# A third PSUM buffer while the pipeline fills, and 512-column products read in 16-column blocks from four 512-byte rows in turn

## What is computed

```python
kv_pool = kv.reshape(B, H // r, r, W // r, r, C).mean(axis=(2, 4))     # B=2, H=384, W=32, C=128, r=4
k = v = kv_pool.reshape(B, -1, C) @ w_sr                               # 768 keys
a = softmax(q @ k.T / sqrt(C))                                         # q: 2 x 12288 x 128
x = a @ v                                                              # attention's output, 24576 rows of 128
h = x @ w1_in;  x = (h * cos(h)) @ w1_out                              # first network, d_ff = 2048
h = x @ w2_in;  x = (h * sigmoid(1.702 * h)) @ w2_out                  # second network, d_ff = 2048
```

## Time and profile before

| | us |
|---|---|
| median of 3 runs | 2718.85 (2718.63 to 2722.79) |
| the profiled execution, its own time | 2722.88 |
| its span, first to last instruction | 2721.1 |
| TensorE (PE) busy | 2670.1 (98%) |
| VectorE (DVE) busy | 2097.1 (77%) |
| GpSimd (POOL) busy | 2029.3 (75%) |
| ScalarE (ACT) busy | 1916.3 (70%) |
| mean granted TensorE clock | 0.993 of 2.4 GHz |

### The profile page before, as it was taken

The page is one execution under the profiler, slowest core; times in us unless marked ns, Lnnn a source line. Parts: engine busy times, 40 slices in busy tenths (PEclk is TensorE's granted clock), DMA queues, the critical chain, the costliest instruction groups (busy, mean ns, idle before and its releaser), DMA issues.

```text
span 2721.1 us, 42506 instructions
## 1 busy us (share of the span) xinstructions
PE 2670.1 (98%) x13342; PEld 2263.0 (83%) x13342; DVE 2097.1 (77%) x2761; ACT 1916.3 (70%) x2471; POOL 2029.3 (75%) x1908
## 2 busy tenths in 40 slices
PE   7999999988999999999999999999999999999998
PEld 7999999966888888888888888888888888888886
DVE  6888888855777777777777777777777777777774
ACT  4777777755777777777777777777777777677775
POOL 2887677547878787778778787777878787777873
PEclk9999999988999999999999999999999999999999
DMA  7323222200000000000000000000000000000000
GB/s 191 72 49 81 71 49 50 50 16 8 10 14 15 8 15 8 15 8 15 13 10 15 8 15 8 15 8 15 15 8 15 8 15 8 15 8 15 16 4 12
DMA packets 220707, 67.64 MB, mean 25 GB/s; under 512 B 204544, under 2 KB 204672, under 8 KB 219776
## 3 DMA queue, kind: packets, MB, share of 16 engines
q1 hardware_dynamic: 220672, 67.21, 10.9%
HBM read 42.01 MB, written 25.17 MB: 25 GB/s over the span
## 4 chain that ended last, share of the span: by engine, by line
PE 96%; DVE 2%; ACT 1%; SPq 0%; DMA 0%; issue 0%; POOL 0%; ACTq 0%
PE psum L548 31%; PE psum L549 30%; PE psum L550 30%; PE psum L672 5%; DVE g L1006 0%; DVE g L1014 0%; ACT turns L835 0%; DMA kv_all<-in_kv 0%; SPq L333 0%; ACT g_hi L845 0%; DVE g_lo L1019 0%; DVE neg_max L926 0%; ACT g L847 0%; PE psum L629 0%; DVE kv_all L892 0%
## 5 line engine op out<-in xcount | busy, mean ns | idle before, releaser
L533 POOL TENSOR_TENSOR g_lo<-g,g_hi 128x512 fp32r<-128x512 f32 x768 | 1122.1, 1461 | 91.0 <-ACT g_hi L852 30.3
L1019 DVE TENSOR_TENSOR g_lo<-g,g_hi 128x1024 fp32r<-128x1024 f32 x384 | 598.3, 1558 | 438.0 <-ACT g L847 432.6
L530 POOL CAST g_hi<-g 128x512 fp32r<-128x512 f32 x758 | 535.1, 706 | 365.2 <-DVE g L1014 365.2
L845 ACT ACTIVATE g_hi<-psum 128x1024 fp32r<-128x1024 f32 x384 | 395.8, 1031 | 440.1 <-PE psum L550 440.1
L548 PE MATMUL psum<-x_hi,w_lo 128*128 128x512 f32 x1536 | 605.2, 394 | 21.1 <-DVE g L1014 21.1
L548 PE MATMUL psum<-g_hi,w_lo 128*128 128x512 f32 x1536 | 600.5, 391 | 9.2 <-DVE x_lo L1025 4.2
L550 PE MATMUL psum<-x_hi,w_hi 128*128 128x512 f32 x1536 | 601.2, 391 | 0.0
L549 PE MATMUL psum<-x_lo,w_hi 128*128 128x512 f32 x1536 | 600.7, 391 | 0.0
L549 PE MATMUL psum<-g_lo,w_hi 128*128 128x512 f32 x1536 | 599.2, 390 | 0.0
L550 PE MATMUL psum<-g_hi,w_hi 128*128 128x512 f32 x1536 | 598.9, 390 | 0.0
L1006 DVE SCALAR_TENSOR_TENSOR g<-turns,psum 128x1024 f32<-128x1024 int32 x384 | 463.0, 1206 | 40.7 <-ACT turns L835 40.7
(11 more groups left out here) (74 smaller groups left out, 3039.0 us busy)
## 6 DMA issues: line engine op xcount, KB each, us to landing
q_blocks<-in_q SPq DMA_DIRECT2D x192, 64.0 KB, 2.2
x_dram<-x_out SPq DMA_DIRECT2D x48, 256.0 KB, 2.3
x_raw<-x_dram SPq DMA_DIRECT2D x48, 256.0 KB, 2.8
out<-y_blocks SPq DMA_DIRECT2D x192, 64.0 KB, 2.3
kv_all<-in_kv SPq DMA_DIRECT2D x4, 1536.0 KB, 11.0
kv_all<-in_kv SPq DMA_DIRECT2D x5, 1024.0 KB, 7.1
w_raw<-in_moe_w_in SPq DMA_DIRECT2D x2, 1024.0 KB, 6.9
kv_all<-in_kv SPq DMA_DIRECT2D x2, 512.0 KB, 9.2
```

What stands on the lines that cost most here:

```text
L530: nc.gpsimd.tensor_copy(g1_hi[p % 4][:, t], g1[p % 4][:, t]).then_inc(g1_hi_ready, 1)
L533: nc.gpsimd.tensor_tensor(g1_lo[p % 4][:, t], g1[p % 4][:, t], g1_hi[p % 4][:, t].bitcast(F32), ALU.subtract).then_inc(g1_lo_ready, 1)
L845: nc.scalar.activation(g2_hi[p % 2][:, :], h2[buffer2(j)], ACT.Silu, scale=GELU)
L1019: nc.vector.tensor_tensor(g2_lo[p % 2][:, :], g2[p % 2][:, :], g2_hi[p % 2][:, :].bitcast(F32), ALU.subtract).then_inc(g2_lo_ready, 1)
```

## The change

It has two parts.

1. **A third `h1` buffer in the filling.** `h1` gets banks 4-5 as a third buffer. For steps below 12 the buffer is `s % 3`, and `up1(s)` waits for `multiply(s - 3)`; from step 12 on it is two buffers as before. `up2(0)`, the first to use banks 4-5 for the second network, now waits until all 12 steps of the filling are multiplied. `BY_SCALAR` becomes 1, 2, 4, 5, 7, 8, 10: ScalarE rounds seven steps of the filling where it rounded five.
2. **The order of the columns in the first network's products.** `up1` and `down1` stream their 512 columns as 8 blocks x 4 rows x 16 columns: 16 columns from each of four rows that lie 128 columns (512 bytes) apart, then the next 16 of each. Output columns in PSUM go the same way, so every number lands where it did. The tiles that are streamed (`x1_*`, `g1_*`) begin 384 bytes behind a multiple of 512 (`APART`), while the weights still begin at a multiple of 512. The second network's and attention's products and places stay as they were.

```diff
     LINE = 512
-    BY_SCALAR = [1, 3, 5, 7, 9]
+    STEP = 16
+    APART = LINE - LINE // 4
+    BY_SCALAR = [1, 2, 4, 5, 7, 8, 10]
...
-    def put(name, shape, dt):
+    def put(name, shape, dt, at=0):
         size = 4 * math.prod(shape[1:])
         if size >= LINE:
-            place[0] += -place[0] % LINE
+            place[0] += (at - place[0]) % LINE
...
-        g1.append(put(f"g1_{n}", [P, PAIR], F32))
+        g1.append(put(f"g1_{n}", [P, PAIR], F32, APART))
...
-    h1 = [banks(0, PAIR), banks(2, PAIR)]
+    h1 = [banks(0, PAIR), banks(2, PAIR), banks(4, PAIR)]
...
+    def buffer1(s, p):
+
+        return s % 3 if isinstance(s, int) and s < UP2 else p % 2
...
+            def by_column_block(x):
+
+                return x.rearrange("p (r b e) -> p b r e", b=LINE // (4 * STEP), e=STEP)
+
+            def product_by_block(dst, w_hi, w_lo, x_hi, x_lo, start, stop):
+
+                return product(by_column_block(dst), w_hi, w_lo, by_column_block(x_hi),
+                               by_column_block(x_lo), start, stop)
+
             def up1(s, p, c):
...
-                if not (isinstance(s, int) and s < 2):
+                if not (isinstance(s, int) and s < UP2):
                     pe.wait_ge(g1_ready, s * 2 - 2)
-                n = p // PAIRS % 2
+                elif s >= 3:
+                    pe.wait_ge(g1_ready, s * 2 - 4)
+                n, at = p // PAIRS % 2, buffer1(s, p)
...
-                    last = product(h1[p % 2][:, k * TOK:(k + 1) * TOK], w1_in_hi[:, f:f + P],
+                    last = product_by_block(h1[at][:, k * TOK:(k + 1) * TOK], w1_in_hi[:, f:f + P],
...
-                    last = product(y1_ps, w1_out_hi[:, f, :], w1_out_lo[:, f, :],
+                    last = product_by_block(y1_ps, w1_out_hi[:, f, :], w1_out_lo[:, f, :],
...
-                elif not (isinstance(j, int) and j == 0):
+                elif isinstance(j, int) and j == 0:
+                    pe.wait_ge(g1_ready, 2 * UP2)
+                else:
                     pe.wait_ge(g2_ready, j)
```

More of the change, by code:

```diff
@@ L137, in attention_and_networks @@
         g1_at = place[0]
-        g1.append(put(f"g1_{n}", [P, PAIR], F32))
+        g1.append(put(f"g1_{n}", [P, PAIR], F32, APART))
         place[0] = g1_at
-        g1_lo.append(put(f"g1_lo{n}", [P, PAIR], F32R))
+        g1_lo.append(put(f"g1_lo{n}", [P, PAIR], F32R, APART))
         place[0] = g1_at
-        turns.append(put(f"turns{n}", [P, PAIR], I32))
-        g1_hi.append(put(f"g1_hi{n}", [P, PAIR], F32R))
+        turns.append(put(f"turns{n}", [P, PAIR], I32, APART))
+        g1_hi.append(put(f"g1_hi{n}", [P, PAIR], F32R, APART))
     x1_raw, x1_lo, x1_hi = [], [], []
@@ L146, in attention_and_networks @@
         x1_at = place[0]
-        x1_raw.append(put(f"x1_raw{n}", [P, TOK], F32))
+        x1_raw.append(put(f"x1_raw{n}", [P, TOK], F32, APART))
         place[0] = x1_at
-        x1_lo.append(put(f"x1_lo{n}", [P, TOK], F32R))
-        x1_hi.append(put(f"x1_hi{n}", [P, TOK], F32R))
+        x1_lo.append(put(f"x1_lo{n}", [P, TOK], F32R, APART))
+        x1_hi.append(put(f"x1_hi{n}", [P, TOK], F32R, APART))
     assert place[0] <= kv_end
@@ L834, in count_turns @@
                 act.wait_ge(h1_ready, i + 1)
-                nc.scalar.activation(turns[p % 4][:, :], h1[p % 2], ACT.Copy, bias=0.25,
+                nc.scalar.activation(turns[p % 4][:, :], h1[buffer1(i, p)], ACT.Copy, bias=0.25,
                                      scale=1.0 / (2 * math.pi)).then_inc(turns_ready, 1)
@@ L1006, in reduce_angle @@
                 nc.vector.scalar_tensor_tensor(g1[p % 4][:, :], turns[p % 4][:, :], -2 * math.pi,
-                                               h1[p % 2], ALU.mult,
+                                               h1[buffer1(i, p)], ALU.mult,
                                                ALU.add).then_inc(angle_ready, 1)
@@ L1013, in multiply @@
                     t = slice(k * TOK, (k + 1) * TOK)
-                    nc.vector.tensor_tensor(g1[p % 4][:, t], h1[p % 2][:, t], g1[p % 4][:, t],
+                    nc.vector.tensor_tensor(g1[p % 4][:, t], h1[buffer1(i, p)][:, t], g1[p % 4][:, t],
                                             ALU.mult).then_inc(g1_ready, 1)
```

## The result

The changed kernel takes 2745.31 us, median of four runs (2744.78 to 2746.19), against 2718.74 for the kernel before in the same comparison: a ratio of 1.0095 (95% interval 1.0078 to 1.0113, written in brackets from here on), slower by 27 us in the medians. The profiled execution took 2746.19, its span is 2744.3.

The account below looks back on a forecast made before the run. The prediction took TensorE's matmul price to bound the steady pipeline and waits the filling. Its terms, -21 (third buffer), -49 (column order) and +4 (second network), sum to -66, from 2718.85 to 2653 us; range 2641 to 2706.

Parts of the forecast that it names:

- What bounds the kernel: Steady pipeline: TensorE busy 500 of 500 us, so a matmul's price is the kernel's; in the filling a wait ends last.
- Part 1, -21 us: Filling: the third buffer removes waits for `multiply`, so `up1(12)` starts earlier; -21 us, bounds -15 (less 1 or 2) to -26.
- that sum: Filling: `up1(12)` starts at 581.1 + 9 x 4.3 = 619.8 us, against 643.5, with two half-clock stretches allowed for.
- Part 2, -49 + 4 us: Steady stretch: new column order makes 4482 first-network matmuls 11 ns cheaper, -49 us; +4 for the second network's disturbed spacing.
- if positions within 512 bytes are what collides, nothing collides any more: First network: stream and weight load stay 384 to about 128 bytes apart in the 512-byte line, never zero.
- the extra of 13.3: Steady pipeline: a 512-column matmul takes 226.7 ns against 213.3 at full clock; the 13.3 ns was called no fixed charge.
- looks like something two reads fight over: TensorE: the matmul's extra 13.3 ns was put on its stream and the next matmul's weight load meeting.
- 11 of 13.3: First network's matmuls: 11 ns of the extra taken as saved, nearest the half-clock rows, leaving 2.
- The bound of +24 us: Part 2's worst side: extra of 19 ns, from 232 ns after a hiccup, over 4482 matmuls; range -60 to +24 us.
- The second network, +4: Its 4608 matmuls keep 226.7 ns, but losing the rhythm costs 25 ns in each of 372 slots: 9 us, half taken.
- Slower: Rival, every `up1` and `down1`: 31 jumps a matmul at one cycle each, 12.9 ns, +58 us, total 2756; chance 0.14.
- The milder form of it: Rival, first network: matmuls stay at 232 ns, +24 - 21, about no change; chance 0.04 for cancelling part 1.

Follow-up runs that it names:

- two rows: Against the changed kernel: first network's streams in 16-column blocks taken in turn from two rows 1024 bytes apart, offset 128 bytes; 2776.89 us (2774.84 at offset 0, 2767.31 at 192).
- the faster pace: Against the changed kernel, with offset 0: first network's columns in two passes, all even blocks of 4 columns, then the odd ones; 2726.20 us.
- the two fine rows: Against the run with two rows 1024 bytes apart: blocks of 4 columns (16 bytes) in place of 16; 2805.48 us.

## Why the prediction was wrong

It gave 2653 us (2641 to 2706); it is 2745. Point by point:

- **What bounds the kernel: right.** A matmul's price in the steady pipeline is the kernel's price; 5 ns on it became some 44 us.
- **Part 1, -21 us: right in the mechanism, the exact figure with some luck.** `up1(2)` at 577.96 (forecast 578), GpSimd's `g_lo` as the main releaser, clock 0.95. `up1(12)` came at 621.6 (forecast 619.8 plus 2 for cold stretches), but not by that sum: the slots took 4.0 us and not 4.3, and the last one 8.5, with the wait of 4.2 us for the first split of the second network's `x`, which the sum left out though the trace of before has it, and with the one cold stretch that was left. The two errors nearly cancel. The run with the buffer alone put part 1 at -19 in its span, and in the filling at -21.2.
- **Part 2, -49 + 4 us: wrong in sign, +42** (the change against the buffer alone; 44 us longer in the steady pipeline, with attention some 1.5 us shorter in this execution). The first network's matmuls went from 226.7 to 235.1 ns, not to 216. The step that failed is "if positions within 512 bytes are what collides, nothing collides any more". Three things in it didn't hold. The places repeat every 256 bytes (offset 256 equals offset 0 in two orders), so the distance of 384 falling to 128 passes through a meeting. But the second thing weighs more: with the period put right, an order meant to keep the reads apart does not help (240 ns at offsets of 0, 128 and 192). That speaks against the extra being the time in which two reads meet, as far as the load goes at the estimated pace of two cycles a column. And the third: the contiguous order was not the costly case that I took it for but as good as any tried. Contiguous or in runs of 256 bytes, with stream and weights at the same place modulo 256 bytes, TensorE holds a beat of 226.7 ns; each other order or distance tried lost it.
- **What I read out of the rows.** That the extra of 13.3 is no fixed charge was right: it is 0 at half clock in the changed order as well (six matmuls from 621.59 to 624.15 above, 426.7 each), 5 to 6 ns more when only the weights move, 26.7 for two rows. That it "looks like something two reads fight over" was half right: relative place counts. But from "it varies" I went to "it can be removed", and took 11 of 13.3 from rows at another clock. The 2 ns that this leaves don't follow from the full-clock rows, which showed 8 at the least, and those of 512 columns off the beat, pointed the other way, to 232. The bound of +24 us that I made of these was too low as well: the first network's matmuls went past 232 to 235.1, +38 us for 4482 of them. That the mean over both networks is 232.0 is a coincidence.
- **The second network, +4: mis-sized.** It is 229 ns instead of 226.7, 2.4 on the mean by part, some 11 us over 4608 matmuls. The mechanism was right: `down2`, right behind `up1`, is off the beat (230.5), and `up2` comes back to it (228.0). A slot loses some 28 ns by it, near the 25 that I took from the earlier trace rows; what failed was the halving, since it happens in every slot.
- **The rivals.** "Slower" came true at a price of 8.4 ns for the first network, but not by its mechanism: a fixed price per jump is refuted. 31 jumps add nothing at offset 384 in the reads alone or in the PSUM writes alone, and 7 in both together nothing at offset 0; in two rows 31 go with 13.3 ns over the beat, and in the faster pace 127 with no more than 4.8. What reads and writes in runs of 16 columns cost together is less clear: 2.5 ns on top of the offset of 384, but 7.5 (`down1`) and 4.3 (`up1`) at offset 0, where no run takes them from their places. The milder form of it, "the beat lost for good at 232", is nearer: the offset alone does that much (231.9 and 233.3). I priced it at +24 for the first network alone.

The Trainium skill ("SBUF — State Buffer", Who interferes with whom) holds that the stream and the weight load have ports of their own and don't wait on anyone. The run with the weights moved by 128 bytes (226.7 to 232.4 ns) disagrees as far as the price goes, since the run with all tiles moved by as much stayed at 226.7: how the two reads lie to each other matters. Whether it is at the ports isn't shown. The Trainium skill ("Advanced Engine Details and Errata", PSUM Cachelines) lets any non-contiguous pattern in PSUM slow matmuls significantly; runs of 16 columns at offset 384 and of 64 at offset 0 did not (231.9 with and without; 226.7 with and without). The dearer ones, runs of 4 columns (231.5 with a gap of 4, 250.0 in two rows) and of 16 at offset 0, don't decide it, since reads and writes jump together there.

**What stays open.** What sets the extra from one matmul to the next isn't settled. It is refuted that it is a sum over the load's columns, a matter of the distance alone, of the pace alone, or of the number of jumps (every 16 columns 240.0 in two rows and 231 to 236 in four; every 4 columns 250 or 231.5). It fits a beat that stream and load have to agree on. At one price the distances are whole multiples of 16 cycles of 2.4 GHz (226.7 ns = 544, 240.0 = 576). Elsewhere they vary, but in several runs they repeat after a few matmuls, and then the sum over one repetition is such a multiple. In `up1` of the change five distances make 1180.0 ns, 2832 cycles (177 x 16), in every slot between 700 and 2600 us:

```profile
1506.16 0.40 PE L554 MATMUL psum<-x_hi,w_lo 128*128 128x512 f32 x1
...
1507.34 0.40 PE L556 MATMUL psum<-x_hi,w_hi 128*128 128x512 f32 x1
```

With the offset alone two distances (237.4 and 229.2 ns) make 1120, with the offset of 64 bytes three make 1648, with that of 32 bytes four make 2240, and in the two fine rows two make 1200. That is an observation, not a shown cause, and the orders without so short a repetition don't test it. No part of any run had a mean under 226.6 ns with 512 columns, so nothing says that any of the 13.3 can be had.

The best version found is the third buffer alone: 2703 us, 0.7% under the kernel before (the runs with all tiles moved, with offset 256 and with blocks of 64 columns, at 2702, are the same within 0.1%). Part 2 should be left out.

## What to carry to other kernels

Where TensorE is the bound and every matmul loads its own weights, keep streams and weights at the same place modulo 256 bytes in SBUF and the stream contiguous (or in runs of 256 bytes): shifting the first network's streams by 32, 64 or 384 bytes, or both networks' weights by 128, cost 1 to 1.7% here, against the same kernel with the buffer alone. An extra that changes with the phase may be the least that there is; before a kernel is built on removing it, measure one order that removes its supposed cause, and take the price of a disturbed beat from the rows where it is disturbed. A pipeline that fills through two PSUM buffers is worth a third, if a bank stands idle meanwhile.

## What was unexpected of the hardware

- The price of a matmul depends on the place of the stream relative to the weight load, modulo 256 bytes: 226.7 ns at 0 and 256, 229 to 234 at 32, 64, 128 and 384 (contiguous; 128 by the weights).
- A stream from two rows in turn, 16 columns each, costs 240.0 ns at offsets of 0, 128 and 192 bytes and whether 128 or 64 weight columns are loaded; in runs of 4 columns 250, though runs of 4 columns in another order cost 231.5.
- Loading 64 weight columns instead of 128 makes contiguous matmuls dearer (230.1 against 226.7), though the load gets shorter.
- At half clock the changed order costs nothing: 426.7 ns, as before.
- Where the distances between matmuls repeat after one to five of them, their sum is a multiple of 16 cycles of 2.4 GHz: 544, 576, 1120, 1200, 1648, 2240, 2832.
- A loss in one network's matmuls spreads to the other's, whose order and places were not touched: 2.4 ns on the mean in the change, 3.8 in `down2`, which in the queue comes right behind `up1`.
